# Second product of a two-layer chain: finished products copied ahead of the next split, the last round's wide sums right behind c12, one load ahead of two stores

## The reference, cut to what matters

```
x = attention(q, k, v), window 64          # 2304 tokens x 512
h = ((x @ w1) * (x @ w2)) @ w3 @ w_out     # 2304 x 512
g = h @ w_in                               # 2304 x 2048, "first product"
g = maximum(0.01 * g, g)                   # leaky
out = g @ w_out2                           # 2304 x 512, "second product"
```

## Time and profile before

| what | value |
|---|---|
| median of three runs | 759.29 us |
| the profiled execution's own time | 758.82 us |
| its span, first to last instruction | 757.0 us |
| PE busy | 742.8 us, 98% of the span |
| VectorE busy | 531.3 us, 70% |
| ScalarE busy | 420.5 us, 56% |
| DMA, mean over the span | 248 GB/s |

### The profile page before, as it was taken

One profiled execution on the slowest core, in us unless ns is written; L12 is line 12 of the kernel. 1 busy time (PEld: TensorE's weight loads), 2 busy tenths in 40 slices (PEclk: granted clock), 3 DMA queues, 4 the chain that ended last, 5 costly groups with the idle time before them and its releaser, 6 DMA issues.

```text
span 757.0 us, 13228 instructions
## 1 busy us (share of the span) xinstructions
PE 742.8 (98%) x4744; PEld 716.5 (95%) x4744; DVE 531.3 (70%) x836; ACT 420.5 (56%) x901; POOL 95.7 (13%) x122
## 2 busy tenths in 40 slices
PE   8999999999999999999999999999998799999998
PEld 7887999999999999999999999999997799999998
DVE  5877988787656768798777968569777555455452
ACT  5876577546564344656646655456674544444441
POOL 3432474414243000000000000000000000000000
PEclk9999999999999999999999999999999899999999
DMA  8884677656863389978858898987996678777731
GB/s 329 318 299 156 228 245 240 199 184 206 272 223 130 127 272 342 340 251 311 307 180 297 308 312 286 352 289 246 386 358 217 213 209 231 214 208 239 210 105 63
DMA packets 97665, 187.39 MB, mean 248 GB/s; under 512 B 8000, under 2 KB 56256, under 8 KB 97600
## 3 DMA queue, kind: packets, MB, share of 16 engines
q1 hardware_dynamic: 91296, 173.57, 69.4%
q10 hardware_dynamic: 6304, 12.98, 4.5%
HBM read 117.31 MB, written 69.21 MB: 246 GB/s over the span
## 4 chain that ended last, share of the span: by engine, by line
PE 74%; DMA 9%; DVE 8%; ACT 3%; issue 3%; SPq 2%; POOL 1%; DVEq 0%; ACTq 0%
PE acc L389 13%; PE acc L391 13%; PE acc L390 13%; PE ps_scores L1644 3%; PE ps_more L389 3%; PE ps_more L391 3%; PE ps_more L390 3%; PE ps_values L1628 2%; PE ps_turned L1636 2%; PE ps_values L389 2%; PE ps_values L391 2%; PE ps_values L390 2%; DMA g_between<-arena 2%; PE ps_scores L389 2%; PE ps_turned L389 2%
## 5 line engine op out<-in xcount | busy, mean ns | idle before, releaser
L1423 DVE TENSOR_TENSOR parts<-arena,parts 128x768 fp32r<-128x768 f32 x72 | 68.7, 958 | 71.0 <-ACT parts L946 71.0
L389 PE MATMUL acc<-parts,weights_b 128*128 128x384 f32 x296 | 100.8, 340 | 4.7 <-ACT arena L866 4.7
L389 PE MATMUL acc<-parts,weights_a 128*128 128x384 f32 (+1 forms) x296 | 103.8, 351 | 0.3 <-DVE arena L1359 0.2
L946 ACT ACTIVATE parts<-arena 128x768 fp32r<-128x768 f32 x72 | 60.7, 847 | 77.9 <-PE acc L391 36.6
L391 PE MATMUL acc<-parts,weights_a 128*128 128x384 f32 (+1 forms) x296 | 101.5, 343 | 0.0
L390 PE MATMUL acc<-parts,weights_a 128*128 128x384 f32 (+1 forms) x296 | 101.4, 342 | 0.0
L391 PE MATMUL acc<-parts,weights_b 128*128 128x384 f32 x296 | 99.7, 337 | 0.0
L390 PE MATMUL acc<-parts,weights_b 128*128 128x384 f32 x296 | 99.6, 337 | 0.0
L827 ACT ACTIVATE arena<-arena,negmax 128x128 f32<-128x128 f32 x144 | 56.0, 391 | 26.8 <-DVE negmax L1208 26.8
L389 PEld LDWEIGHTS acc<-parts,weights_b 128*128 128x128 f32 x296 | 56.1, 190 | 5.1 <-DVE parts L1423 5.0
L389 PEld LDWEIGHTS acc<-parts,weights_a 128*128 128x128 f32 x296 | 55.9, 189 | 3.5 <-DVE arena L1359 0.8
(11 more groups left out here) (236 smaller groups left out, 1880.8 us busy)
## 6 DMA issues: line engine op xcount, KB each, us to landing
g_between<-arena SPq DMA_DIRECT2D x77, 384.0 KB, 4.8
arena<-g_between SPq DMA_DIRECT2D x77, 384.0 KB, 3.7
arena<-qk_steps SPq DMA_DIRECT2D x36, 512.0 KB, 4.4
arena<-p_between SPq DMA_DIRECT2D x42, 384.0 KB, 5.0
arena<-v_steps SPq DMA_DIRECT2D x36, 256.0 KB, 3.1
p_between<-arena SPq DMA_DIRECT2D x24, 384.0 KB, 5.5
x_between<-arena ACTq DMA_DIRECT2D x21, 384.0 KB, 5.5
arena<-x_between SPq DMA_DIRECT2D x21, 384.0 KB, 5.2
```

The source lines that it names most:

```text
L389: eng.matmul(out_ap, w_hi, m_hi, start=start, stop=False, skip_group_check=resumed)
L946: act.activation(block_places[k % NPROD][:, 0:BW].rearrange("p (j t) -> p j t", j=2), t_source(k), ACT.Copy).then_inc(t_hi, 1)
L1423: dve.tensor_tensor(lo, t_source(k), hi.bitcast(F32), ALU.subtract).then_inc(t_lo, 1)
```

## The change

ScalarE, in the second product's loop: the copies that become due with item k - 7 now stand ahead of `split_t(k)`, no longer behind it. VectorE, in the last round (r = 26): both wide sums stand right behind `make_c12`, ahead of items 4 to 6 and the last two fills; before, they stood behind item 6. VectorE also takes the two parts of fill 25 ahead of item 2 instead of behind it. SP, in round h = 10: the load of item 3 is issued between the third and the fourth group of stores, ahead of two store DMAs, instead of behind them.

```diff
# SP
                 if h == HR - 1:
-                    load_t(3)
                     load_fill(late)
                     load_t(4)
                     load_fill(late + 1)
...
                 store_g(r, 2)
+                if h == HR - 2:
+                    load_t(3)
                 store_g(r, 3)
# ScalarE
             for k in range(TROUND + 2, TB + NPROD):
-                if k < TB:
+                if k < NPROD:
                     split_t(k)
-                if k < NPROD:
                     continue
...
                             if c == NC2 - 1:
                                 store_last(s)
+                if k < TB:
+                    split_t(k)
                 if step == 1:
# VectorE
                 make_c22(r, s)
-            split_t(2)
             split_fill(NFILL - 3, 0)
             split_fill(NFILL - 3, 1)
+            split_t(2)
             split_t(3)
             for s in range(2):
                 make_c12(r, s)
+            g_sums13(r, 0)
+            g_sums13(r, 1)
             for f in (NFILL - 2, NFILL - 1):
                 split_t(4 + f - NFILL + 2)
                 split_fill(f, 0)
                 split_fill(f, 1)
             split_t(6)
-            g_sums13(r, 0)
-            g_sums13(r, 1)
             split_t(7)
```

## The result

The changed kernel took 755.4 us (median of six runs, 753.04 to 756.2) against 759.36 us for the kernel before on the same chip (six runs): ratio 0.9937, 95% interval 0.9918 to 0.9957, that is 3.3 to 6.2 us less. The ratio is that of the means (755.03 to 759.79, 4.8 us apart); the medians lie 4.0 us apart. The forecast was 754.3, in a range from 751.8 to 757.0.

The account below looks back on a forecast made before the run. TensorE was taken to bound the second product except in its first steps; 4.28 us at item 8 plus (2.35 - 1.6) of clock made 5.0 off 758.82, 753.8, or 754.3 on the median's scale; range 751.8 to 757.0.

Parts of the forecast that it names:

- The wide sums: VectorE, last round: both sums behind `make_c12` fall in idle time, item 7's wait goes, item 11's load goes earlier; 2.8 us.
- The copies ahead of the split: ScalarE, second product: copies of P1 pass two splits after item 11 instead of three; 0.74 us gained.
- Item 8's start: PE: item 8 starts at 589.15 instead of 593.43, 4.28 us earlier, after a remaining wait of 2.75 us.
- The clock: TensorE around item 8: the clock still falls, slow matmuls cost an estimated 1.6 us instead of 2.35.
- The forecast case: Whole chain with a clock fall at item 8: 5.0 us off, 754.3 us; chance 0.47.
- rival 1: Item 8: same chain but no clock fall, 6.6 us off, 752.7 us; chance 0.3.
- The load of item 3: SP queue: issued ahead of two stores, item 3 ready about 1.5 us earlier; bounds no gain and 1.6 us.
- Item 4: PE: only its load binds, so it starts at 576.21 instead of 576.95, its wait gone; 0.74 us gained.
- PE's distances 2.87 and 2.87 stay: PE, items 4 to 5 and 5 to 6: distances unchanged, with waits of 0.52 and 0.51 us.
- Rival 4: DMA queue: fill 27 and pushed stores delay item 4's load; 3.1 us slower, 762.4 us; chance 0.04.
- Sum: Whole change: 4.28 us at item 8 plus (2.35 - 1.6) from the clock, 5.0 us off.

## Why the prediction was right, and where it was not

- *The wide sums* (2.8 us): right. They ran in idle time, item 7 lost its wait, the load of item 11 went earlier; alone they gave 2.9 (1.7 to 3.7).
- *The copies ahead of the split* (0.74): right by the trace, 0.64 from item 7 to item 8 with this part alone, and no wait appears later. In time alone 0.8, which the interval doesn't part from no change.
- *Item 8's start* (4.28 earlier, a wait of 2.75): 4.24 earlier from item 0, a wait of 2.84.
- *The clock* (a fall, 1.6 lost): 1.57 in the profile, in part by luck. The forecast case and rival 1 are both true: of the six runs four show a mean clock of 0.998 and 755.1 to 756.2 us, two show 1.000 and 753.04 and 754.26. The reasoning did not hold. A fall was taken because a wait of 2.75 is close to the 2.8 us after which the clock fell before; but from item 7's last matmul to the fall went 3.6 us here, 2.3 with the wide sums only and 4.1 with the copies only, so 2.8 was no fixed delay. And no row gave 1.6: it was said to be less than 2.35 because matmuls begin as the clock falls, but a low stretch as long as the one before (591.54 to 598.4), all of it under matmuls, would have cost more (half of it, an estimate of 3.4). It cost less because the low stretch was shorter (591.2 to 594.6). By the Trainium skill (TensorE: Matmul & The Clock Gate, section on HAM oscillation) bursts behind waits start slow; here four of six executions of one program show the fall, and in the profile the burst began fast and turned slow 0.8 us in.
- *The load of item 3*: its size was off. Its high part came 2.5 us earlier from item 0 (571.08 - 567.74 = 3.34 before, 569.76 - 568.95 = 0.81 after), beyond the bound of 1.6: the issue came 1.6 earlier and the flight was 0.9 shorter. The shorter flight is not shown to come from the order: in the seven other profiles with this order the high part starts 0.8 to 1.9 after item 0, and flights of 5.1 to 6.3 us there overlap the 5.5 to 6.2 of the old order. In the changed kernel it did not bind, as item 4's own load does.
- *Item 4* (0.74 gained): at item 4 0.89 was gained, at item 5 0.78. The step "PE's distances 2.87 and 2.87 stay" failed: item 4 to item 5 took 2.98, because item 5's load, which the prediction took to be there, landed 0.63 after ScalarE wanted it. As item 4 came 0.15 earlier than forecast, item 5 started almost where it was forecast (11.30 after item 0, 11.34 forecast). The miss was small in the whole change, but most of the term in the kernel with this part alone (1.0003).
- *Item 3 and `make_c12`*: the prediction has no term for the 0.13 us by which `make_c12` was ahead of item 3. The kernel without the load and fill order shows it at work (0.68 us of wait).
- *Rival 4* (item 4 overtaken): item 4's load flew 575.13 - 570.09 = 5.0 us, less than before. No overtaking was seen.
- *Sum*: 5.0 against 4.95 from item 0 to item 13. The median came 1.1 us above the forecast; the profiled execution came 1.3 above its own (753.8), of which 1.2 was lost ahead of the changed stretch.

## What to carry to other kernels

The view of waits names who ends a wait, not what to move: here it named a copy; moving the copy past one split was worth some 0.7 us by the trace, and moving two sums that had stood ready for eight microseconds 2.9. Follow the wait back until an instruction stood ready with nothing missing but its turn, and then look again at the queue of the last releaser: moving two copies past a load-bound split took 3.6 us more, where the whole change had taken 4.8 (by the ratios). A wait on TensorE should be priced with the clock behind it, and a gain behind a full DMA queue only up to the next load's landing.

## What the runs showed of the hardware that was not expected

The price of a fall of the clock does not follow the length of the wait. Waits of 4.72, 4.63, 4.05, 3.62, 2.85, 2.84, 2.83 and 2.64 us lost 2.35, 2.20, 1.58, 2.60, 1.58, 1.57, 1.47 and 1.41 us; waits of 1.6 us and less lost none. What it follows in these profiles is how long matmuls ran while the clock was low: about half of that time is lost (4.9 us before, 3.4 in the changed kernel).

One program shows more than one price. The profiles that lost 2.2 us or more have a mean clock of 0.995 or 0.996, those that lost 1.4 to 1.6 have 0.998. Of the 41 executions of the kernel before that ran beside the experiments, 30 show 0.995 or 0.996 and 11 show 0.998; the changed kernel shows 0.998 in four and 1.000 in two. So one profile does not give the price of a wait, and differences of about 1 us between two kernels can be the clock's. In the changed kernel the fall came when matmuls had been running again for 0.8 us (item 8 at 590.40, the first slow one at 591.17).

The flight of one and the same kind of load (384 KB) was 3.1 to 3.5 us with an idle queue (item 11) and 4.7 to 6.6 us with a full one (items 3 to 5), and in the full queue it moved by more than 1 us between executions.
